# The second mixing of each chunk goes into its own chunk's first slots, and wv's low parts go from GpSimd to VectorE

## What is computed

```python
def _attn_ref(q, k, v, p):                      # 8 x 8 heads x 576 x 64, p has 32 rows
    p_packed = sm_attn(p, k, v)
    out = sm_attn(q, p_packed, p_packed)
...
def _moe_ref(x, mu_k, mu_r, w_k, w_v, w_r):     # x: 8 x 576 x 512, w_k 512 x 1024
    x_prev = np.concatenate([np.zeros((B, 1, D)), x[:, :-1, :]], axis=1)
    xk = mu_k * x + (1.0 - mu_k) * x_prev
    xr = mu_r * x + (1.0 - mu_r) * x_prev
    k = np.maximum(xk @ w_k, 0.0)
    v = k * k @ w_v
    r = 1.0 / (1.0 + np.exp(-(xr @ w_r)))
    return r * v
...
def _moe2_ref(x, U, V, w_ch1, w_ch2):           # w_ch1 512 x 2048
    h = x.transpose(0, 2, 1) @ U @ V
    u = x + h.transpose(0, 2, 1)
    return u + np.maximum(u @ w_ch1, 0.0) @ w_ch2
```

## Time and profile before

| | us |
|---|---|
| three timed runs | 1340.59, 1338.31, 1340.4; median 1340.4 |
| the profiled execution, its own time | 1340.01 |
| its span, first to last instruction | 1338.2 |
| PE busy | 1304.4 (97%) |
| DVE busy | 957.9 (72%) |
| ACT busy | 697.1 (52%) |
| POOL busy | 233.5 (17%) |
| mean granted TensorE clock | 0.993 |

### The profile page before, as it was taken

One profiled execution on the slowest core, in us unless ns is written; L12 is line 12 of the kernel. 1 busy time (PEld: TensorE's weight loads), 2 busy tenths in 40 slices (PEclk: granted clock), 3 DMA queues, 4 the chain that ended last, 5 costly groups with the idle time before them and its releaser, 6 DMA issues.

```text
span 1338.2 us, 21378 instructions
## 1 busy us (share of the span) xinstructions
PE 1304.4 (97%) x7626; PEld 1128.1 (84%) x7626; DVE 957.9 (72%) x1557; ACT 697.1 (52%) x1233; POOL 233.5 (17%) x328
## 2 busy tenths in 40 slices
PE   7899999999999999999999999999999999999997
PEld 6768888878888888888999999888888888888886
DVE  5977978786878777774568676857587566857557
ACT  4657556456555555544546554645355534645353
POOL 3702132324142103511002003000030003000000
PEclk9999999999999999999999999999999999999999
DMA  9646595839384614965888899787757886678766
GB/s 241 160 76 107 124 177 128 161 101 175 81 173 106 156 24 123 286 189 132 276 271 253 271 267 314 237 248 218 233 187 197 258 225 213 192 207 215 220 194 136
DMA packets 431577, 252.57 MB, mean 189 GB/s; under 512 B 311536, under 2 KB 350480, under 8 KB 431472
## 3 DMA queue, kind: packets, MB, share of 16 engines
q1 hardware_dynamic: 414768, 232.31, 65.4%
q0 software_dynamic: 10096, 17.78, 4.9%
q10 hardware_dynamic: 6608, 1.11, 0.5%
HBM read 201.25 MB, written 49.81 MB: 188 GB/s over the span
## 4 chain that ended last, share of the span: by engine, by line
PE 75%; DVE 5%; SPq 4%; DMA 3%; issue 1%; ACT 1%; POOL 0%; DVEq 0%; ACTq 0%
PE bank L1178 25%; PE bank L1264 24%; PE bank L923 9%; PE bank L909 8%; PE bank L888 5%; SPq L1450 2%; DMA w_ring<-w_parts 1%; SPq L1588 1%; PE bank L1005 1%; PE bank L1077 1%; PE bank L713 1%; DMA kq_parts<-in_q 0%; DMA x_scratch<-x 0%; DVE square L972 0%; DVE x2s_lo L1016 0%
## 5 line engine op out<-in xcount | busy, mean ns | idle before, releaser
L1178 PE MATMUL bank<-u_parts,w_ring 128*128 128x512 f32 (+1 forms) x1680 | 353.7, 368 | 1.1 <-DVE hid_raw L1223 1.1
L1264 PE MATMUL bank<-hid_parts,w_ring 128*128 128x512 f32 (+1 forms) x1680 | 349.5, 368 | 1.2 <-DVE acc L1312 0.5
L1264 PEld LDWEIGHTS bank<-hid_parts,w_ring 128*128 128x128 f32 x1680 | 304.9, 188 | 44.2 <-issue 3.8
L1178 PEld LDWEIGHTS bank<-u_parts,w_ring 128*128 128x128 f32 x1680 | 304.9, 188 | 40.9 <-issue 1.8
L1287 ACT ACTIVATE hid_parts<-hid_raw 128x512 fp32r<-128x512 f32 (+1 forms) x280 | 164.7, 588 | 134.6 <-PE bank L1264 133.8
L1293 DVE TENSOR_TENSOR hid_parts<-hid_raw,hid_parts 128x512 fp32r<-128x512 f32 (+1 forms) x280 | 180.8, 646 | 63.5 <-ACT hid_parts L1287 59.0
L909 PE MATMUL bank<-xk_hi,wk_hi 128*128 128x384 f32 x384 | 132.1, 344 | 1.9 <-DVE x L983 1.9
L909 PE MATMUL bank<-xk_lo,wk_hi 128*128 128x384 f32 x384 | 129.5, 337 | 0.0
L909 PE MATMUL bank<-xk_hi,wk_lo 128*128 128x384 f32 x384 | 129.3, 337 | 0.0
L923 PE MATMUL bank<-wv_hi,k_hi 128*128 128x512 f32 x288 | 113.5, 394 | 0.0
L923 PE MATMUL bank<-wv_lo,k_hi 128*128 128x512 f32 x288 | 112.2, 390 | 0.0
(11 more groups left out here) (176 smaller groups left out, 1937.1 us busy)
## 6 DMA issues: line engine op xcount, KB each, us to landing
w_ring<-w_parts SPq DMA_DIRECT2D x560, 256.0 KB, 3.7
w_parts<-early_out SPq DMA_DIRECT2D x23, 896.0 KB, 5.0
x_scratch<-x SPq DMA_DIRECT2D x144, 64.0 KB, 2.1
kq_parts<-in_q SPq DMA_DIRECT2D x112, 72.0 KB, 2.9
...
```

Source lines behind the costliest of these rows:

```text
L1178: last = nc.tensor.matmul(to, wring[:, e % RW, ct, a, :], uc[:, pos, b, ct, 0:w], start=(pos in FRESH and ct == 0 and a == 0 and b == 0), ...
L1264: last = nc.tensor.matmul(role(st, j, BANK_OF[pos])[:, 0:w], wring[:, e % RW, j, a, :], hid[:, no % RH, b, 0:w], start=(pos in FRESH and i ...
```

## The change

Five things are done in `chunk_plan` and around it.

1. The second mixing of chunks 2 to 11 moves. Before, `mix` 1 stood beside slot v0b of the chunk before and `split` 1 beside v1b (beside k3 of its own chunk where that is the first of a pair). Now `mix` 1 stands beside k2 and `split` 1 beside k4 of its own chunk, in all chunks but 0; chunk 1 had it so before.
2. `x2s` of the second tile stands ahead of slot k0 instead of behind it.
3. In MIDDLE and LAST, `norm1` of a pair's second batch moves from the last slot of the pair before to slot k0, `outA` from k2 to k3 (`outB` stays beside k4); in chunks 5 and 8 `pp` moves from k6 to k7 and `scores2` from r0 to r1. In chunk 0 `pv` with `qA` moves from k4 to k5, and `qB` from k5 to k6. Some pieces move by a slot or a few.
4. The low parts of wv (four tiles) are made by VectorE, one instruction of 1024 columns each: one before chunk 0 and three beside its slots k0, k5 and k7. GpSimd keeps wr's two tiles.
5. The waits follow: the second split of chunk 0 waits for wr's two and two of wv's tiles, its first sigmoid for three and its second for four.

```diff
-EARLY, FIRST_AT, EARLY_AT = 20, (23, 31, 38, 43), (1, 6, 11, 15, 27, 31, 35, 39)
+EARLY, FIRST_AT, EARLY_AT = 20, (23, 33, 39, 44), (1, 6, 11, 15, 27, 31, 36, 41)
+WV_LO_AT = (0, 5, 7)
...
-        fourth = batch_slots(32, 33, 35, 37, 38, 39, 40, 42, 45, 47, 50, 53, 55)
+        fourth = batch_slots(32, 33, 35, 37, 38, 39, 41, 43, 45, 47, 51, 54, 55)
...
-        second = {0: ("scores1",), 2: ("a",), 4: ("pv", "qA"), 5: ("qB",), 8: ("pp",), 9: ("scores2",),
+        second = {0: ("scores1",), 2: ("a",), 5: ("pv", "qA"), 6: ("qB",), 8: ("pp",), 9: ("scores2",),
...
+        if at == 0 and (c > 0 or kind != FIRST):
+            items.append(("x2s", 7 if c == 0 else 3 * c - 2, -1 if c == 0 else 0))
         items.append(slot)
...
-            at0 = (15, 15) if kind == FIRST and c == 0 else MIX_AT if c < 2 else MIX_AT[:3]
+            at0 = (15, 15) if kind == FIRST and c == 0 else MIX_AT[:2]
...
-        if kind == FIRST and c == 1 and at in (2, 4):
-            items.append(("mix" if at == 2 else "split", 1, 1))
-        if kind != FIRST and c == 0 and at == 3:
-            items.append(("split", 1, 0))
+        if (kind != FIRST or c > 0) and at in (2, 4):
+            items.append(("mix" if at == 2 else "split", 1, c))
...
-    items += [("attn", 1, "p"), ("load_p", 2)]
+    items += [("attn", 1, "p"), ("load_p", 2), ("wv_lo", 0)]
...
-            act.wait_ge(w_lo, NWA - CT - 2)
+            act.wait_ge(wr_lo_ok, CT // 2)
+            act.wait_ge(wv_lo_ok, 2)
...
-        for i in range(CT, NWA):
+        for i in range(CT, CT + CT // 2):
...
+            elif item[0] == "wv_lo":
+                i = NWA - CT + item[1]
+                dve.wait_ge(w_hi, i + 1)
+                _, dst, a = w_chunks[i]
+                nc.vector.tensor_tensor(dst[1], parts(stage_a[i % RA], a), dst[0].bitcast(F32),
+                                        ALU.subtract).then_inc(wv_lo_ok, 1)
```

More of the change, by code:

```diff
@@ L140, in chunk_plan @@
             behind = -1 if c == 0 else 0
-            if at == 0:
-                items.append(("x2s", 7 if c == 0 else 3 * c - 2, behind))
-            elif at == 2:
+            if at == 2:
                 items.append(("g", 7, 1, -1) if c == 0 else ("g", 3 * c - 2, 0, 0))
@@ L174, in chunk_plan @@
             items.append(("w", NWA - 2 if at == 2 else NWA - 1))
+        if kind == FIRST and c == 0 and at in WV_LO_AT:
+            items.append(("wv_lo", WV_LO_AT.index(at) + 1))
         if kind == FIRST and c == 0 and at == 6:
@@ L217, in first_items @@
     items += [("mix", 0, 0), ("split", 0, 0), ("k1",)] + [("w", i) for i in range(nw, NWA - 2)]
-    items += [("attn", 1, "p"), ("load_p", 2)]
+    items += [("attn", 1, "p"), ("load_p", 2), ("wv_lo", 0)]
     return items
 def piece_items():
-    plan = {6: [("ws_load", EARLY + m) for m in range(SLOTS_P + 1)]}
+    plan = {4: [("ws_load", EARLY + m) for m in range(SLOTS_P + 1)]}
     for m in range(PIECES - EARLY):
@@ L490, in build @@
     w_in = [sem(f"w_in{i}") for i in range(RA)]
-    w_hi, wk_lo_ok, w_lo = sem("w_hi"), sem("wk_lo_ok"), sem("w_lo")
+    w_hi, wk_lo_ok, wr_lo_ok, wv_lo_ok = sem("w_hi"), sem("wk_lo_ok"), sem("wr_lo_ok"), sem("wv_lo_ok")
     scaled_prev, mix_ok, x_hi, x_lo = sem("scaled_prev"), sem("mix_ok"), sem("x_hi"), sem("x_lo")
@@ L953, in act_group @@
                 act.wait_ge(u_split, 1)
-                act.wait_ge(w_lo, NWA - CT)
+                act.wait_ge(wv_lo_ok, 3)
+            if isinstance(C, int) and C == 0 and at == 1:
+                act.wait_ge(wv_lo_ok, 4)
             ge(act, x2s_lo, TPC * (C - 1) + at + 1)
@@ L1693, in _ @@
                                                dst[0][:, :, own].bitcast(F32), ALU.subtract)
-            last.then_inc(w_lo, 1)
+            last.then_inc(wr_lo_ok, 1)
             if i + RA < NWA:
-                pool.wait_ge(w_lo, i - CT + 1)
+                pool.wait_ge(wr_lo_ok, i - CT + 1)
                 load_w(i + RA)
@@ L1755, in do_a @@
                         pe.wait_ge(wk_lo_ok, CT)
+                    elif item[0] == "r":
+                        pe.wait_ge(wr_lo_ok, CT // 2)
                     else:
-                        pe.wait_ge(w_lo, {"r": CT // 2, "v": NWA - CT}[item[0]])
+                        pe.wait_ge(wv_lo_ok, CT)
                 pe_group(pe, C, c, item)
@@ L1885, in do_a @@
             C = CHUNKS * g + c
-            if item[0] == "u_prep":
+            if item[0] in ("u_prep", "wv_lo"):
                 first(item)
```

2 lines of the change are left out of this document (1 added, 1 removed).

## The result

The changed kernel takes 1356.8 us (median of 4 runs, 1355.4 to 1357.4) beside 1339.8 us before: ratio 1.0139, 95% interval 1.0121 to 1.0156. It is slower by 17 us. The forecast was 1352.5 with 1341 to 1359. The profiled execution took 1356.3 us with a span of 1354.5; before, 1340.0 and 1338.2.

A forecast was written before the change was run, and what follows sets the result against it. PE, busy 97% of the span, was taken as the bound in phase A. The terms -5.4 - 2.9 - 2.0 + 6.4 + 6.8 + 0.8 + 2.8 + 6.0 gave +12.5 on 1340.0: 1352.5 us, range 1341 to 1359.

The forecast's parts named there:

- Chunk 0: VectorE, freed from slow running beside GpSimd, makes packedT 4.1 us sooner; PE gains 4.0 and the clock 1.4: -5.4 us.
- Chunk 2: PE's 1.9 us wait for L983 and its slow clock go (-3.6), later pT costs +0.7: -2.9 us.
- Chunks 3, 6, 9: outB: outB waits for VectorE's later copy of outA: 2.5 us in chunks 3 and 6, 1.4 in 9, sum +6.4.
- Chunks 4 and 7: r0: r0 waits for the second split, delayed behind scores2's exponential on ScalarE: 3.4 us each, +6.8 us.
- Chunks 5 and 8: Mixing and split ahead of `packed` raise PE's wait from 1.3 to about 1.7 us: +0.8 for both.
- Chunk 10: The 1.1 us wait for `x2s_lo` goes since pieces come sooner; with chunk 3's 0.9, -2.0 us.
- Chunk 11: SP's loads wait for the chunk's own mixing and go 6.8 us later, so acc comes late: +2.8 us.
- Clock: Granted clock falls behind four new stalls, in chunks 3, 4, 6 and 7, at 1.5 us each: +6.0 us.
- The rival on the faster side: VectorE's slack absorbs the moves in chunks 3 to 9, outB and r0 do not wait: -7.5, 1333 us; chance 0.11.

The follow-up runs named there:

- e1: Kernel before with only wv's low parts on VectorE, pv and qA beside k5 and qB beside k6: 1335.6 us, ratio 0.9980.
- e7: Kernel before with only pv and qA beside k5 and qB beside k6 in chunk 0, wv left on GpSimd: 1339.6 us, ratio 1.0015.
- e6: Changed kernel with outB beside k5 instead of k4 in chunks 3, 6 and 9: 1347.4 us, ratio 1.0084 to the kernel before.
- e10: Changed kernel once more, without an edit, giving its second profile: 1357.9 us, ratio 1.0149 to the kernel before.
- e2: Changed kernel with second mixing beside k1 and its split beside k3 in chunks 4 and 7: 1349.2 us, ratio 1.0082 to the kernel before.
- e5: Changed kernel with chunks 3 to 11's second mixings and norm1, outA, outB put back as before: 1330.4 us, ratio 0.9949 to the kernel before.
- e3: Changed kernel with chunk 10's second mixing alone back in chunk 9: 1352.8 us, ratio 1.0112 to the kernel before.
- e4: Changed kernel with chunk 11's second mixing alone back in chunk 10: 1353.0 us, ratio 1.0113 to the kernel before.
- e8: Changed kernel with mixing and split beside k1, k3 in chunks 4 and 7, outB beside k5, mixings of chunks 10 and 11 put back: 1340.4 us, ratio 1.0018.

## Why the prediction was right, and where it was not

It was right in sign, in mechanism for the larger terms, and within 4.3 us of the median. That it came so close is in part luck: chunks 10 and 11 cost 5.6 us more than forecast and chunks 3, 5, 7 and 8 together 4.1 less, and the clock fell in four chunks of which two were named. The steps, in its own order:

- **Chunk 0 (-5.4 forecast, -4.6 measured with what lies ahead of it).** The mechanism holds (e1, e7). GpSimd's end at 52.4 instead of about 66 us let the squares behind it take 0.55 to 0.56 us (one 0.82). Over-sized was what PE could get back: 1.5 us of packedT's wait stayed and 0.9 of the one for v's rows, where I had said that the first comes under 1 us and the second goes. packedT came 2.6 us sooner (29.1 us after k0 instead of 31.7), not 4.1. I had let the relief begin at 49.89 us, where GpSimd began on wv before; but its work on wr now lasted until 52.4, and until then a square still took 1.09 us (0.58 before) and the mixing 3.17 instead of 2.17. These are the missing 1.5 us. In the second profile the clock fell behind packedT's wait and the gain of the chunk was 2.6 us.
- **Chunk 2 (-2.9, measured -2.3).** L909's wait went with its slow clock, and the new one for pT is 1.1 us where I gave 0.7.
- **Chunks 3, 6, 9: outB (+2.5, +2.5, +1.4).** Shown, by the copy's time in chunk 6 (14.1 us after k0 for 14.4), and by e6, in which chunks 6 and 9 lose it again. In chunk 3 it is right in place, but its size hangs on a store that VectorE waits for (e10).
- **Chunks 4 and 7: r0 (+3.4 each).** Shown by the row at r0 and by e2; the waits were 1.2 and 2.1 us in both chunks, 3.3 together. ScalarE's exponential in the same queue was the right reason.
- **Chunks 5 and 8 (+0.4 each): wrong in sign**, -0.7 and -0.4. I set mixing and split (4.0) against a piece (1.1) and one slot (2.1). By these terms the wait of 1.3 becomes 2.1 and not 1.7; it became 0.5 and 0.9. In e5, without the mixing, it is 0 and 0.3, so mixing and split made PE's wait some 0.5 us longer and not 4.0; the rest was slack that the sum had left out.
- **Chunk 10: the step that failed.** The prediction counted "The waits for `x2s_lo` of 0.9 and 1.1 go" and "in chunk 10 the pieces come sooner". The wait there grew from 1.1 to 2.5 us and the chunk by 2.8. In chunk 3 the wait went, as forecast. In chunk 10 I had looked at the pieces alone, and not at the mixing that now stands beside k2 while GpSimd works on a piece. e3 shows that the mixing costs 3.3 us in all, and the rows show how: it slows GpSimd, the piece ends 12.5 us after k0 instead of 11.2, ScalarE waits for it, and the tile's low part comes 3.08 us after its end as in every profile. Without the mixing the piece does come sooner (10.7), and that half of the sentence is right.
- **Chunk 11 (+2.8, measured +4.5).** The loads' time was right to 0.4 us. The late loads alone cost 1.6 to 1.9 us (e4 against e2, e3 and e10); the rest of the 4.5 is 1.3 us of a slower landing and some 1.5 of slow clock in that one profile. The prediction's 5.9 us to landing was a median of two loads, the second of them in phase B. The one that acc waits for took 5.0 us in the kernel before, and with 5.0 the sum gives 1.9 us. That the waits of the first profile add up to 3.0, near the 2.8, is luck.
- **Clock (+6.0 for chunks 3, 4, 6 and 7).** In the first profile the granted clock was below 1.00 in chunks 4, 6, 10 and 11 and at 1.00 in 3 and 7. In the second it fell in 0, 3, 6 and 10 and was 1.00 in 4, 7 and 11. Four stalls paid in the first, as counted, but not the four named. The Trainium skill, "TensorE: Matmul & The Clock Gate", section "HAM oscillation — how this bites in real kernels", says of a kernel that waits about 3 to 5 us for DMA in every pass that its array is throttled in every pass. The waits here are mostly shorter, and it is not certain behind which of them the clock falls. The wait at r0 of 2.1 us was in both chunks 4 and 7, and the clock of the one was 0.97 and of the other 1.00. The 2.3 us at outB in chunk 6 had it fall in four profiles and not in e2. In chunk 3 the waits of 4.0 to 5.0 us had it fall each time (e2, e3, e4, e10), as the Trainium skill has it for such waits, and the one of 3.0 did not.

The rival on the faster side (VectorE's slack takes the moves) fell with the first row of waits. e8 shows how near it lay: with the order mended, the mixings of chunks 10 and 11 put back, and wv's gain included, the same idea ends 0.2% from the kernel before.
